# Attention values in two alternating groups of 64 stationary columns

## The reference

```python
scores = scale * np.matmul(q, k.transpose(0, 1, 3, 2))
thresh = np.max(scores, axis=-1, keepdims=True) - tau
scores = np.where(scores >= thresh, scores, -1000000000.0)
scores = scores - np.max(scores, axis=-1, keepdims=True)
attn = np.exp(scores)
attn = attn / (np.sum(attn, axis=-1, keepdims=True) + 1e-09)
out = np.matmul(attn, v)
# x = out as (2304, 512)
# first mixture: 8 experts, argmax of x @ w_gate chooses one per token,
#   gate * (relu(x @ w1[e]) @ w2[e])
# second mixture: 4 experts, all of them for every token,
#   sum over e of p[:, e] * (relu(x @ w1[e]) @ w2[e])
```

## Time and profile before

| | |
|---|---|
| time, median of 3 runs (1532.12 to 1532.68) | 1532.43 us |
| time of the profiled execution | 1532.18 us |
| its span, first to last instruction | 1530.4 us |
| mean granted TensorE clock | 0.988 |
| TensorE busy (9200 matmuls) | 1484.4 us, 97% |
| VectorE busy | 792.2 us, 52% |
| ScalarE busy | 640.8 us, 42% |
| matmuls of L590 | 1600, from 20.9 to 366.3 us |

### The profile page before, as it was taken

One profiled execution on the slowest core, in us unless ns is written; L12 is line 12 of the kernel. 1 busy time (PEld: TensorE's weight loads), 2 busy tenths in 40 slices (PEclk: granted clock), 3 DMA queues, 4 the chain that ended last, 5 costly groups with the idle time before them and its releaser, 6 DMA issues.

```text
span 1530.4 us, 25432 instructions
## 1 busy us (share of the span) xinstructions
PE 1484.4 (97%) x9200; PEld 1365.8 (89%) x9200; DVE 792.2 (52%) x1310; ACT 640.8 (42%) x1328; POOL 149.9 (10%) x274
## 2 busy tenths in 40 slices
PE   7999999999389999999999999999999999999999
PEld 7999999998288888889999999999999999999998
DVE  6888888887767777776422224222242222432222
ACT  5787778776156666665222223111131111321111
POOL 2111111111011122220100000000000000000000
PEclk9999999999699999999999999999999999999999
DMA  5344434442278888897300003000030000100001
GB/s 118 87 101 94 105 92 99 94 104 55 88 234 273 273 278 275 285 313 250 128 1 1 1 0 110 0 1 1 1 98 14 1 0 1 56 21 21 22 21 42
DMA packets 169700, 143.90 MB, mean 94 GB/s; under 512 B 96256, under 2 KB 140384, under 8 KB 169632
## 3 DMA queue, kind: packets, MB, share of 16 engines
q1 hardware_dynamic: 160560, 120.37, 27.1%
q0 software_dynamic: 6640, 21.97, 4.1%
q10 hardware_dynamic: 2432, 0.59, 0.2%
HBM read 111.56 MB, written 16.12 MB: 83 GB/s over the span
## 4 chain that ended last, share of the span: by engine, by line
PE 90%; DVE 5%; issue 2%; DMA 1%; ACT 1%; SPq 0%; DVEq 0%; ACTq 0%
PE S L731 11%; PE S L733 11%; PE S L732 11%; PE bank L744 9%; PE bank L746 9%; PE bank L745 9%; PE S L590 8%; PE S L626 5%; PE bank L639 3%; PE S L745 3%; PE S L746 3%; PE S L744 3%; DVE pr L1014 2%; DMA ring<-in_moe_w 1%; PE S L565 1%
## 5 line engine op out<-in xcount | busy, mean ns | idle before, releaser
L894 ACT ACTIVATE hth<-S 128x384 fp32r<-128x384 f32 (+1 forms) x264 | 121.5, 462 | 676.2 <-PE S L733 673.7
L731 PE MATMUL S<-xch,wh 128*128 128x384 f32 (+1 forms) x1056 | 339.8, 322 | 5.2 <-DVE xcl L1208 4.4
L733 PE MATMUL S<-xch,wl 128*128 128x384 f32 (+1 forms) x1056 | 339.4, 321 | 0.0
L732 PE MATMUL S<-xcl,wh 128*128 128x384 f32 (+1 forms) x1056 | 339.3, 321 | 0.0
L1214 DVE SCALAR_TENSOR_TENSOR htl<-S,hth 128x384 fp32r<-128x384 f32 (+1 forms) x264 | 136.8, 520 | 289.4 <-ACT hth L894 289.2
L744 PE MATMUL bank<-wh,hth 128*128 128x512 f32 x584 | 229.7, 393 | 2.5 <-DVE htl L1228 2.5
L746 PE MATMUL bank<-wh,htl 128*128 128x512 f32 x584 | 228.0, 390 | 0.0
L745 PE MATMUL bank<-wl,hth 128*128 128x512 f32 x584 | 227.8, 390 | 0.0
L1200 DVE TENSOR_TENSOR wl<-ring,wh 128x1024 fp32r<-128x1024 f32 x160 | 191.4, 1223 | 55.2 <-ACT wh L885 54.3
L731 PEld LDWEIGHTS S<-xch,wh 128*128 128x128 f32 x1056 | 200.3, 190 | 7.4 <-DVE xcl L1208 4.8
L732 PEld LDWEIGHTS S<-xcl,wh 128*128 128x128 f32 x1056 | 200.2, 190 | 1.2
(11 more groups left out here) (204 smaller groups left out, 1877.8 us busy)
## 6 DMA issues: line engine op xcount, KB each, us to landing
ring<-in_moe_w SPq DMA_DIRECT2D x160, 512.0 KB, 4.7
raw<-in_k SPq DMA_DIRECT2D x36, 128.0 KB, 2.4
tokens_x<-x_nat SPq DMA_DIRECT2D x16, 288.0 KB, 5.0
x_nat<-compact_y POOLq DMA_DIRECT2D x6, 768.0 KB, 7.7
raw<-in_q SPq DMA_DIRECT2D x34, 128.0 KB, 3.1
vv<-in_v SPq DMA_DIRECT2D x34, 128.0 KB, 2.2
qb<-qa SPq DMA_DIRECT2D x16, 224.0 KB, 3.2
qa<-qb SPq DMA_DIRECT2D x16, 224.0 KB, 3.5
```

Source lines behind the costliest of these rows:

```text
L731: pe.matmul(hb(f, n), w1_block(wh, kk, f), xch[:, kk, 0:n], start=kk == 0, stop=False)
L732: pe.matmul(hb(f, n), w1_block(wh, kk, f), xcl[:, kk, 0:n], start=False, stop=False)
L733: last = pe.matmul(hb(f, n), w1_block(wl, kk, f), xch[:, kk, 0:n], start=False, stop=kk == KD - 1)
L894: act.activation(hth[:, f, 0:n], hb(f, n), ACT.Relu).then_inc(s_hh, 1)
```

## The change

The values of every tile are computed in two groups of 64 stationary columns. The loop over the key blocks is now outside and the one over the halves inside, so the groups alternate; each half writes its own 64 PSUM partitions. The operands and the results are the same. For a full tile both halves use the same `vv`; for the middle tile each uses its batch's.

```diff
             def values(j, slot):
 
                 bp, t = j // QT, j % QT
-                last = None
-                for b in range(2):
-                    if (b == 0 and t > MID) or (b == 1 and t < MID):
-                        continue
-                    lo, hi = (0, P) if t != MID else (b * HALF, (b + 1) * HALF)
-                    for kb in range(KB):
-                        last = pe.matmul(ob(slot, lo, hi), pt[j % 3][:, kb, lo:hi], vv[bp][:, b, kb, :],
+                for kb in range(KB):
+                    for half in range(2):
+                        lo = half * HALF
+                        b = half if t == MID else int(t > MID)
+                        last = pe.matmul(ob(slot, lo, lo + HALF), pt[j % 3][:, kb, lo:lo + HALF], vv[bp][:, b, kb, :],
                                          start=kb == 0, stop=kb == KB - 1)
                 return last
```

## The result

The changed kernel takes 1516.12 us (median of 4 runs, 1515.61 to 1516.47) against 1532.28 for the one before on the same chip: a ratio of 0.9895 with a 95% interval of 0.9878 to 0.9912. The forecast was 1520.8, in a range of 1509 to 1542; 11.4 us were foreseen and 16.2 came. The profiled execution took 1516.2 us, 16.0 less than the profiled one before, and all of that lies ahead of the last values' matmul. This is the line of the values' matmuls in the kernel after (duration min/median/max in ns, then the first and last start): the last one starts at 350.3 where it was 366.3. The first starts at 20.3 where it was 20.9, so 0.6 of the 16.0 us was won before any values were multiplied; in the other kernels here it starts anywhere from 20.3 to 20.9. From the first to the last values' matmul it is 15.5 us less.

The account below looks back on a forecast made before the run. TensorE was taken to set the pace in 7.63 us of each 21.88 us window, tied with VectorE in the other 14.25. 15 x 0.70 plus 0.86 us gave 11.4 us off 1532.2: 1520.8 us, range 1509 to 1542.

Parts of the forecast that it names:

- The halves run together: Values' matmuls: alternating 64-column halves overlap throughout, each stream keeping its 0.057 us spacing; forecast held at 62%.
- the serial rival: Values' matmuls: alternating halves don't overlap, a full tile takes 1.72 us and the kernel 1579 us; chance 15%.
- The price of going in and out: Around each tile's values: every tile pays the middle tile's 0.20 us in and 0.16 us out.
- The new length: A tile's 20 values' matmuls, first to last start: 0.64 us, so a full tile saves 0.13, the middle one 0.34.
- perfect overlap: Lower end of the range for a tile's 20 values' matmuls: 0.58 us, or 1.17 us with the steps in and out.
- three tiles count and six are swallowed: Attention window: three tiles in TensorE's 7.63 us stretch save 0.60 us; the other six's 0.78 us is mostly swallowed.
- VectorE's gaps: VectorE's busy 14.25 us stretch of each window: of 0.56 us idle, 0.10 us can close.
- The last five tiles: End of the last window, middle tile and four more with nothing of VectorE beside them: 0.86 us saved.
- TensorE's new idle time: Ahead of the transposes in the first stretch, waiting for the mask: some 0.7 us a window.
- the 20.8: Attention window: falling below 20.8 us with TensorE's idle time small would refute what is late next; 21.2 us was expected.
- rival 3: Attention window: VectorE isn't the limit, so all nine tiles count, 1.38 us a window, 1510 us; chance 8%.
- the layers behind attention stay as they were: After the attention stage: the layers start earlier and are otherwise as before.

Follow-up runs that it names:

- six-tile kernel: Only the six tiles other than 4, 5 and 6 alternate halves, those three as in the kernel before: 1532.00 us, ratio 1.0002 against the kernel before.

## Why the prediction was right, and where its size was off

**The halves run together.** Right. Five loads in flight in the middle tile's seam was the evidence, four to six is what all tiles show after. The rule of the Trainium skill that weight loads run beside matmuls in flight only where the row groups differ ("TensorE: Matmul & The Clock Gate", Part 3, The mechanism) would have ended at the serial rival, 1579 us; no run came near it, and even with one half wholly before the other (1552.28) the seam still overlaps. What this case shows for column groups on all 128 rows is four to six loads in flight against two.

**The price of going in and out.** Right: 0.20 and 0.15 us, the middle tile's, now in every tile. A full tile had 0.11 in and 0.08 out, so the form costs 0.16 us, nearly as much again as a full tile saves.

**The new length.** This is the term that was mis-sized. I took 0.64 us, with 0.06 for the second half to start behind the first; it starts at once and the length is 0.58, the end that I had called perfect overlap. A full tile saves 0.19 and the middle one 0.40, not 0.13 and 0.34. With three tiles a window that is 2.7 us in 15 windows, of the 4.6 us that the sum missed in the profiled execution.

**What reaches the end.** The split was right. I said that three tiles count and six are swallowed; alone they bring 12.0 and 3.7 us. In the window: 0.40 + 2 x 0.19 = 0.78 from the three tiles, 0.13 from VectorE's gaps (0.10 foreseen), and 0.06 where the stretches meet: before, TensorE began the transposes at 204.83, 0.17 after the mask's end, and after at 196.35, 0.06 after it, but takes 0.05 longer to the last of them. That is the 0.97 between 21.88 and 20.91, and 14.5 us in 15 windows. The 0.27 a window that I missed are 0.18 of length, 0.03 of gaps and 0.06 at that seam. The first tiles bring 0.1 us and the earlier start of the first values 0.6, which has nothing to do with the change and which I hadn't in the sum.

The last five tiles bring 0.87 us (358.49 to 366.35 before, 343.33 to 350.31 after), and I had 0.86, but by luck. I had said that nothing of VectorE lies beside them. Yet two of them start the next values after 1.79 and 1.67 us in both kernels and save nothing, because the transposes behind them wait, as in

```profile
346.45 0.66 PE L637 MATMUL bank<-ident,pr 128*128 128x128 f32 x4 [0.30 <-DVE pr L1012]
```

and the others save more than I had foreseen.

**What would be seen.** TensorE's new idle time is there, nearly all of it where I named it, in the wait for the mask: 14.4 us more on the weight loads. Once a window it also waits 0.13 us ahead of the values for VectorE's split of q and k (1.8 us in all), which I had overlooked. Together that is about what the six tiles save and don't bring to the end, 15 x (6 x 0.19 - 0.13) = 15 us. The window fell to 20.91, just above the 20.8 at which I would have had to give up VectorE as the bound; rival 3 (1510 us) is refuted by the six tiles' 3.7 us.

**The rest.** That the layers behind attention stay as they were holds for the changed kernel: first matmul of the first expert to the end is 1105.8 us in both. It isn't certain in general, as the six-tile kernel shows with 1111.7.

## What to carry to other kernels

Where a short moving operand (65 columns of f32 here) meets 128 stationary columns, try splitting the stationary columns into halves that take turns at every accumulation step. Runs of two steps gave 13 of the 16 us here, runs of three only 6, and a full half at a time was 20 us slower than not splitting. Other types and widths weren't measured. Look in the old trace for a place where the new neighbourhood already occurs, if only once, and count what is in flight there. Then sum only the tiles that stand where the engine sets the pace, and look for what the next engine could do elsewhere: moving two small VectorE instructions out of its busy stretch was worth a quarter of the whole change. And watch the length of the loop: with twice the instructions for the values its code was fetched anew in every pass, and the gain was lost twice over.

## What the runs showed that I had not expected

- 40 loads and 40 matmuls of 32 columns went through in 0.56 us from first to last start, 0.014 us a pair; with 64 columns it was 0.58 for 20. In both the pairs of one group stay some 0.057 us apart, and ten of them in a row are what the length consists of.
- A loop body with 720 pairs for the values stood still 3.3 to 4.0 us behind each of its six jumps back, and 46 instruction packets of 16 KB came from 100 to 340 us; with 360 or 480 pairs there was no standstill and no packet.
- Standstills of 1 to 2.4 us occur in the expert stages of some kernels whose code there is the same (6.3 us in the six-tile kernel's profile, two of the three with no wait behind them). They swallowed a gain of 3.7 us; where they come from stays open.
- A wait of a weight load that the trace puts down to VectorE (11.3 us in all) was the way into the 64-column form in all but 1.8 us: the same 0.17 us stood before the tiles where nothing is named.
- After a maximum that followed the divisors at once, the mask began 0.67 us after its start; in the same step without them 0.79.
